# The first output projection of a three-stage attention and MLP kernel, written as seven half-size products for pairs of token tiles

## The reference

```python
x = attention(q, k, v)                 # windowed, 2304 tokens x 512
h = max(x @ w1, x @ w2, x @ w3)        # 512 -> 768
y = h @ w_out                          # 768 -> 512, the step that the change rewrites
z = y @ w_in2                          # 512 -> 2048
g = where(z >= 1, z, where(z <= -1, 0, (z + 1)**2 / 4))
return g @ w_out2                      # 2048 -> 512
```

## Time and profile before

| what | value |
|---|---|
| three timed runs | 748.75, 748.91 and 750.69 us, median 748.91 |
| the profiled execution | 749.52 us, its span in the trace 747.7 us |
| granted TensorE clock | 1.000 as mean of the core |
| busy PE / PEld / DVE / ACT / POOL | 740.5 / 657.0 / 300.4 / 330.3 / 313.8 us |

### The profile page before, as it was taken

One profiled execution on the slowest core, in us unless ns is written; L12 is line 12 of the kernel. 1 busy time (PEld: TensorE's weight loads), 2 busy tenths in 40 slices (PEclk: granted clock), 3 DMA queues, 4 the chain that ended last, 5 costly groups with the idle time before them and its releaser, 6 DMA issues.

```text
span 747.7 us, 12711 instructions
## 1 busy us (share of the span) xinstructions
PE 740.5 (99%) x4731; PEld 657.0 (88%) x4731; DVE 300.4 (40%) x744; ACT 330.3 (44%) x795; POOL 313.8 (42%) x239
## 2 busy tenths in 40 slices
...
PEclk9999999999999999999999999999999999999999
...
DMA packets 24040, 46.18 MB, mean 62 GB/s; under 512 B 2224, under 2 KB 3632, under 8 KB 23984
## 3 DMA queue, kind: packets, MB, share of 16 engines
...
q10 hardware_dynamic: 432, 0.49, 0.2%
...
## 4 chain that ended last, share of the span: by engine, by line
PE 98%; DVE 1%; DMA 0%; ACT 0%; issue 0%; SPq 0%; DVEq 0%
PE wide L540 30%; PE wide L619 26%; PE bank L599 24%; PE wide L572 10%; PE wide L502 3%; PE bank L526 3%; PE bank L511 2%; PE wide L547 1%; DVE part_in L965 0%; DMA q<-q_dram 0%; ACT prob L641 0%; DVE prob L849 0%; ACT pT L656 0%; SPq L416 0%; DVE xT L836 0%
## 5 line engine op out<-in xcount | busy, mean ns | idle before, releaser
L540 PE MATMUL wide<-xT,w 128*128 128x512 f32 (+1 forms) x1080 | 234.7, 373 | 0.0
L540 PEld LDWEIGHTS wide<-xT,w 128*128 128x128 f32 x1080 | 186.3, 188 | 34.7 <-issue 2.1
L619 PE MATMUL wide<-w4s,gT 128*128 128x512 f32 x864 | 205.6, 391 | 0.0
L619 PEld LDWEIGHTS wide<-w4s,gT 128*128 128x128 f32 x864 | 161.3, 188 | 32.1 <-POOL gT L1016 0.4
L1016 POOL TENSOR_TENSOR gT<-g,gT 128x384 fp32r<-128x384 f32 x96 | 111.6, 1173 | 175.1 <-ACT gT L636 175.1
L599 PE MATMUL bank<-yT,w3s 128*128 128x384 f32 x1008 | 183.6, 336 | 0.0
L599 PEld LDWEIGHTS bank<-yT,w3s 128*128 128x128 f32 x1008 | 177.2, 188 | 4.1 <-DVE g L957 0.3
L939 DVE TENSOR_TENSOR pu<-bank,pu 128x384 f32<-128x384 f32 x72 | 40.1, 557 | 174.8 <-PE bank L599 172.9
L1024 POOL TENSOR_TENSOR prob<-prob,row_inv 128x512 f32<-128x512 f32 x36 | 38.2, 1064 | 153.6 <-DVE row_inv L855 153.6
L762 ACT ACTIVATE g_sq<-g_sq,half 128x384 f32<-128x384 f32 x96 | 58.9, 616 | 85.4 <-DVE g_sq L951 83.4
L869 DVE TENSOR_TENSOR h<-wide,h 128x512 f32<-128x512 f32 (+1 forms) x60 | 38.0, 634 | 94.9 <-PE wide L540 94.8
...
## 6 DMA issues: line engine op xcount, KB each, us to landing
...
```

Source lines behind the costliest of these rows:

```text
L540: mm = pe.matmul(acc[gr % 2][:, 0:cols], w123[:, wp, w, kc, c * P:(c + 1) * P], xT[:, x_side(t), xp, kc, 0:cols], start=(kc == x == 0), st ...
L619: mm = pe.matmul(acc4[b], gT[:, k, gp, tb * P:(tb + 1) * P], w4s[pair_f(g) % HALF_F][:, wp, f, :], start=(first and x == 0), stop=(last an ...
```

## The change

Layer 2 takes pairs of token tiles (three pairs, `TILE_PAIRS`) and goes by the scheme of layer 3: the contraction of 768 is cut in halves of three pieces (`KH`), the 512 outputs in halves of two chunks (`j`), and seven products stand in for eight. A product is, for each `j`, 9 matmuls of 384 columns. Seven data operands per pair (`h_op0` to `h_op6`, each of 1152 elements per partition) replace `h1s`; four of them (2 to 5) are new sums made by DVE (`sum_of_h`, four instructions a pair, `first_sums` and `late_sums`, one in place in `h1`). Seven weight operands replace the two of `wo1`, with four new sums and all parts on POOL. Results gather in four banks; ACT copies three of the four outputs of each `j` (`l2_copy`, then `l2_last` for the last), DVE adds the other products to the copies (`l2_add`). The remainders of operands 5 and 6 of later pairs go to POOL, between the weight parts of layer 3. Layer 3's weight loads start when two operands of the first pair are done; its data operands `yT` (which now lie where `h_op2` to `h_op6` lay, in part) are made during the last pair.

```diff
+    if engine == "DVE":
+        at = LAYER1_AT[-1]
+        later += [(at + 8.2, "h_low", 0), (at + 9.2, "h_low", 1), (at + 13.2, "h_sum", 0), (at + 14.2, "h_sum", 1),
+                  (at + 15.2, "h_sum", 2)]
...
-    wo1, at = place("wo1", [P, 2, C1, DM], F32R, A_AT)
-    h1s, H1S_END = place("h1s", [P, 2, 2, C1, MTOK], F32R, at)
-    RAW_AT = H1S_END + 4 * MTOK // 3
+    wo1, at = place("wo1", [P, 2, PRODUCTS, KH, 2 * P], F32R, A_AT)
+    h_ops = [None] * PRODUCTS
+    for m in range(2):
+        h_ops[m], at = place(f"h_op{m}", [P, 2, KH, MTOK], F32R, at)
+    for m in range(2, PRODUCTS):
+        h_ops[m], _ = place(f"h_op{m}", [P, 2, KH, MTOK], F32R, A_AT - 4 * 2 * KH * MTOK * (PRODUCTS - m))
+    wo1_sums, end = place("wo1_sums", [P, 2, KH, 2 * P], F32, X_AT + 4 * 2 * KC * MOST)
+    assert end <= A_AT
+    RAW_AT = at + 4 * MTOK // 3
...
+            late_sums, _ = place("late_sums", [P, 2, KH, MTOK], F32, at - W4_BYTES)
+            t_sums, at = place("t_sums", [P, 3, 2, MTOK], F32, at)
...
+    def l2_banks(t, j):
+        two = p_ps if j == 0 else acc4
+        return two[(t + 1) % 2], two[t % 2]
...
+    def h_operand(t, m):
+        return {0: h_half(t, 0, 0), 1: h_half(t, 1, 0), 2: h_sums(t)[:, 1, :, :], 3: h_sums(t)[:, 0, :, :],
+                4: h_half(t, 0, 1), 5: h_sums(t)[:, 1, :, :], 6: h_half(t, 1, 1)}[m]
...
-        sp.wait_ge(wo1_lo, 1)
+        sp.wait_ge(h_lo[3], 1)
+        sp.wait_ge(h_lo[5], 1)
...
-        pe.wait_ge(wo1_lo, 1)
-        with pe.Fori(0, MTILES) as t:
-            for c in range(KC):
-                pe.wait_ge(y_out, KC * t + c - 1 + Y_CREDIT)
-                if c < 2:
-                    pe.wait_ge(acc_free[c], GROUPS // 2 * L1_TILES + ACC_CREDIT)
-                if c == 0:
-                    pe.wait_ge(h1_lo, t + 1)
-                for kc in range(C1):
-                    for x, (wp, hp) in enumerate(PASSES):
-                        mm = pe.matmul(acc[c % 2][:, 0:MTOK], wo1[:, wp, kc, c * P:(c + 1) * P],
-                                       h1s[:, of(t, 1), hp, kc, :].rearrange("p a n -> p (a n)"),
-                                       start=(kc == x == 0), stop=(kc == C1 - 1 and x == 2))
-                mm.then_inc(l2_done, 1)
+        def layer2(t, m, j):
+            a, c = l2_banks(t, j)
+            if j == 0:
+                pe.wait_ge(h_lo[m], t + 1)
+            if t == m == j == 0:
+                pe.wait_ge(wo1_lo, PRODUCTS)
+            if m == 0:
+                after(pe, l2_added, 6 * (t - 1) + 4 + j + 1)
+            elif m == 1:
+                after(pe, l2_out, 2 * (t - 1) + j + 1)
+            elif m == 2:
+                pe.wait_ge(l2_copied, 6 * t + j + 1)
+            elif m == 3:
+                pe.wait_ge(l2_added, 6 * t + j + 1)
+            elif m == 4:
+                pe.wait_ge(l2_copied, 6 * t + 2 + j + 1)
+            elif m == 5:
+                pe.wait_ge(l2_copied, 6 * t + 4 + j + 1)
+            else:
+                pe.wait_ge(l2_added, 6 * t + 2 + j + 1)
+            bank = c if m in (1, 3, 5) else a
+            for kc in range(KH):
+                for x, (wp, hp) in enumerate(PASSES):
+                    mm = pe.matmul(bank[:, 0:MTOK], wo1[:, wp, W_OF[m], kc, j * P:(j + 1) * P], h_ops[m][:, hp, kc, :],
+                                   start=(m in (0, 1, 3) and kc == x == 0), stop=(kc == KH - 1 and x == 2),
+                                   skip_group_check=True)
+            mm.then_inc(l2_made, 1)
+        for t in range(TILE_PAIRS):
+            for m in range(PRODUCTS):
+                for j in range(2):
+                    layer2(t, m, j)
...
+                if g == 0:
+                    pe.wait_ge(l2_added, 6 * TILE_PAIRS - 1)
...
-        def h1_parts(t):
-            hi(h1s[:, of(t, 1), 0, :, :].rearrange("p a c n -> p (a c) n"), h1[:, :, ds(t * MTOK, MTOK)])\
-                .then_inc(h1_hi, 1)
-        def y_chunk(t, c):
-            act.wait_ge(l2_done, KC * t + c + 1)
-            act.activation(h1[:, c, t * MTOK:(t + 1) * MTOK], acc[c % 2][:, 0:MTOK], ACT.Copy).then_inc(y_out, 1)
+        def h_high(t, m):
+            if t > 0:
+                act.wait_ge(l2_made, 2 * PRODUCTS * (t - 1) + 2 * (m + 1))
+            if m in (2, 3, 4, 5):
+                act.wait_ge(h_sum, 4 * t + (3, 1, 2, 4)[m - 2])
+            hi(h_ops[m][:, 0, :, :], h_operand(t, m)).then_inc(h_hi[m], 1)
+        def l2_copy(t, n):
+            if n == 0:
+                act.wait_ge(h_sum, 4 * t + 2)
+            elif n == 1:
+                act.wait_ge(h_sum, 4 * t + 4)
+            else:
+                act.wait_ge(h_lo[4], t + 1)
+                act.wait_ge(h_lo[6], t + 1)
+            for j in range(2):
+                act.wait_ge(l2_made, 2 * PRODUCTS * t + 2 * (0, 2, 3)[n] + j + 1)
+                act.activation(y_chunk(t, j, (0, 2, 1)[n]), l2_banks(t, j)[(0, 0, 1)[n]][:, 0:MTOK], ACT.Copy).then_inc(l2_copied, 1)
+        def l2_last(t):
+            for j in range(2):
+                act.wait_ge(l2_made, 2 * PRODUCTS * (t + 1) - 1 + j)
+                act.activation(y_chunk(t, j, 3), l2_banks(t, j)[0][:, 0:MTOK], ACT.Copy).then_inc(l2_out, 1)
...
-        with act.Fori(0, 1) as t:
-            h1_parts(t)
+        h_high(0, 0)
+        h_high(0, 1)
         for b in range(2):
             act.wait_ge(acc_free[b], GROUPS // 2 * L1_TILES + ACC_CREDIT)
-        for t_at in range(MTILES):
-            if t_at + 1 < MTILES:
-                h1_parts(t_at + 1)
-            for c in range(KC):
-                y_chunk(t_at, c)
-                at = KC * t_at + c - 1
-                if 0 <= at < 8:
-                    j, part = divmod(at, 4)
-                    if part < 3:
-                        w3_parts(j, part)
-                    else:
-                        w4_parts(j)
-                elif 10 <= at < 10 + PRODUCTS:
-                    if at == 10:
-                        act.wait_ge(y_out, 2 * KC + Y_CREDIT)
-                    y_part(0, at - 10)
-        act.wait_ge(y_out, KC * MTILES + Y_CREDIT)
+        for m in (2, 3, 4, 6):
+            h_high(0, m)
+        for t in range(TILE_PAIRS):
+            more = t + 1 < TILE_PAIRS
+            l2_copy(t, 0)
+            if t == 0:
+                h_high(0, 5)
+            if more:
+                h_high(t + 1, 0)
+                h_high(t + 1, 1)
+            l2_copy(t, 1)
+            if t == 1:
+                w4_parts(0)
+            elif t == 2:
+                act.wait_ge(l2_added, 6)
+                w4_parts(1)
+                y_part(0, 0)
+            if more:
+                h_high(t + 1, 2)
+            l2_copy(t, 2)
+            if more:
+                h_high(t + 1, 3)
+            else:
+                y_part(0, 1)
+            if t < 2:
+                w3_parts(t, 0)
+                w3_parts(t, 1)
+            if more:
+                h_high(t + 1, 4)
+                h_high(t + 1, 5)
+                w3_parts(t, 2)
+            else:
+                for m in (2, 3, 4):
+                    y_part(0, m)
+            l2_last(t)
+            if more:
+                h_high(t + 1, 6)
+        y_part(0, 5)
+        y_part(0, 6)
+        act.wait_ge(l2_added, 6 * TILE_PAIRS)
...
+        def sum_of_h(t, n):
+            b11, b12, b21, b22 = (h_half(t, k, tile) for k in range(2) for tile in range(2))
+            t3, t2 = (h_sums(t)[:, i, :, :] for i in range(2))
+            if n == 0:
+                if t == 0:
+                    dve.wait_ge(wo1_lo, PRODUCTS)
+                elif t == 1:
+                    for b in range(2):
+                        dve.wait_ge(acc_free[b], GROUPS // 2 * L1_TILES + ACC_CREDIT)
+                else:
+                    dve.wait_ge(h_lo[3], t)
+                dve.tensor_tensor(t3, b22, b12, ALU.subtract).then_inc(h_sum, 1)
+            elif n == 1:
+                dve.wait_ge(h_sum, 4 * t + 1)
+                dve.tensor_tensor(b12, b12, b11, ALU.subtract).then_inc(h_sum, 1)
+            elif n == 2:
+                dve.wait_ge(h_sum, 4 * t + 2)
+                if t == 2:
+                    dve.wait_ge(h_lo[5], t)
+                dve.tensor_tensor(t2, b22, b12, ALU.subtract).then_inc(h_sum, 1)
+            else:
+                dve.wait_ge(h_lo[2], t + 1)
+                dve.tensor_tensor(t2, b21, t2, ALU.subtract).then_inc(h_sum, 1)
+        def l2_add(t, n):
+            for j in range(2):
+                dve.wait_ge(l2_made, 2 * PRODUCTS * t + 2 * (1, 4, 5)[n] + j + 1)
+                dve.wait_ge(l2_copied, 6 * t + 2 * (0, 2, 1)[n] + j + 1)
+                to = y_chunk(t, j, n)
+                dve.tensor_tensor(to, l2_banks(t, j)[(1, 0, 1)[n]][:, 0:MTOK], to, ALU.add).then_inc(l2_added, 1)
...
-        weight_sums(0)
-        h1_low(1)
-        h1_low(2)
-        weight_sums(1)
-        dve.wait_ge(y_out, 2 * KC + Y_CREDIT)
+        h_low(0, 2)
+        sum_of_h(0, 3)
+        h_low(0, 3)
+        h_low(0, 4)
+        l2_add(0, 0)
+        h_low(0, 5)
```

(72 more changed lines are left out.)

40 lines of the change are left out of this document (22 added, 18 removed).

## The result

The changed kernel takes 755.92 us, median of 4 runs (755.4 to 757.15), against 748.83 for the kernel before (748.29 to 750.69): ratio 1.0089, 95% interval 1.0075 to 1.0102. It is 7.1 us **slower**, where +6.1 was forecast. The profiled execution took 755.4 us, its span is 753.4.

What follows compares the result with a forecast made beforehand. TensorE was taken as the bound, busy 99% without gaps. Saved matmuls of -9.4 us and seven waits of +15.4 gave +6.1 after rounding, a forecast of 755.0 us, with a range of 749.5 to 761.0.

Steps and rivals of the forecast that it cites:

- The saving: Layer 2 on PE: 378 matmuls in place of 432, 54 x 173.4 ns, 9.4 us less.
- all seven: Seven places in layer 2 and at layer 3's start where PE waits for late operands, copies or adds: together 15.4 us.
- What costs nothing: POOL's weight work, SP's later loads, the first two products' operands and most ACT copies come before PE needs them: 0 us.
- waits 1 to 5 and 7: PE in layer 2's pairs: 1.3, 1.2, 3.1, 1.3 and 3.5 us; at layer 3's product 3: 3.3 us.
- Waits 3 and 5: Product 1 of pairs 1 and 2 waits for ACT's last copy: 3.1 and 3.5 us, 3.0 each with no POOL.
- wait 3: Pair 0 to 1, product 1: PE waits for `l2_last`, behind the weight sums' high part on ACT: 3.1 us.
- The collisions: DVE and POOL both at work on SBUF: each waits out the other's whole instruction; without this the sum is 2.8 us faster.
- wait 7: Layer 3, product 3: first add stands behind four DVE weight sums taking turns with POOL's last `yT` remainders: 3.3 us.
- Wait 6: Layer 3, product 0: DVE's last layer 2 adds stand behind a data sum and POOL's `yT` remainder: 1.8 us.
- wait 5: Pair 1 to 2, product 1: PE waits for ACT's last copy behind the weight sums' high part: 3.5 us.
- The clock: Rival, chance 0.10: PE's clock falls to 1.2 GHz after long waits, 4.5 us a fall, 759.5 to 768.5 us.

Runs made afterwards that it cites:

- kernel 5: The kernel before with 54 of layer 2's 432 matmuls left out, all else as it was: 739.04 us, ratio 0.9873.
- Kernel 3: The changed kernel with POOL writing zeros in place of its remainders from layer 2's start to layer 3's start: 747.38 us, ratio 0.9978 to the kernel before.
- Edit 6: The changed kernel with five remainders of operands 5 and 6 moved from POOL to DVE: 753.06 us, ratio 1.0058 to the kernel before.
- kernel 4: The changed kernel with 20 unused matmuls ahead of each of the three products that wait longest: 754.2 us, ratio 1.0072 to the kernel before.

## Why the prediction was right, point by point

**The saving**: 54 x 173.4 ns = 9.4 counted, 9.3 measured (kernel 5).

**The places of the waits**: all seven stand where they were put, and nowhere else did PE wait in layers 2 and 3. *What costs nothing* held: POOL's last weight remainder ended at 273.7, over 19 us before PE needed it, and no wait ahead of layer 2 or in it was for the weights or the late loads.

**The sizes of waits 1 to 5 and 7**: 13.7 forecast, 12.8 measured, each a little short. Waits 3 and 5 came 0.2 to 0.3 shorter. The parts that the prediction lists for wait 3 add up to 9.65 us with its 0.1 a hand-over, not to the 9.4 it goes on with. Measured from the end of product 5 (314.38) to 323.50 it was 9.12: on DVE one remainder started before the one ahead of it had ended, so that the chain has two in 2.54 and not 2 x 1.36. Kernel 3 shows what they rest on: with no POOL reads they are 2.8 by the table's measure, not 3.0.

**The collisions**: the rule of the prediction (each waits out the other's whole instruction) gave DVE's sums at layer 3's start and wait 7 at 3.3; measured 3.11. Kernel 3 took the reads away and wait 7 with them. Edit 6, which only moves work off POOL, gained 2.4.

**Wait 6**, the term most off: 1.8 forecast, 0.64 measured. The remainder of `yT` that it hangs on ended where it was forecast, within 0.3 us once layer 1's 1.2 us are allowed for (367.8 against 369.2); PE came later, since the clock had fallen behind wait 5 (kernel 4: without that fall it is 1.64).

**The clock, the step that failed.** It was a rival (C, chance 0.10) and not a term of the sum. It did fall, twice, and that was the rival's own sign, a granted clock under 1 behind a wait. What the rival had wrong was the price: 4.5 us a fall, taken from the kernel's first 9 us, where a fall cost 1.5. Nor does a row show that those 9 us were a fall: in the trace of the kernel before their matmuls are slow (16 in 1.13 us at 4.60, 16 in 0.67 at 11.28), but the view of the granted clock says 1.00 from 4.60 to 11.50. The page "TensorE: Matmul & The Clock Gate" of the Trainium skill (HAM oscillation — how this bites in real kernels) says that long idle gaps throttle the engine; the windows at 0.51 and 0.50 agree. It should have stood in the forecast itself, at the price of one short stretch.

So two errors ran against each other: the seven terms, which add up to 15.5 and not 15.4, were 2.1 too long, and 3.6 for the clock and the restarts was left out. That the forecast of +6.1 came so near to +7.1 is in part luck.
